# A chunked delta-rule attention kernel with two feed-forward stages: two halves of the key products of every second step made in one go, and the router's ranks moved ahead of the last solve

## The reference

```python
def _attn_ref(q, k, v, beta):              # (4, 8, 768, 48)
    k_n = k / (np.linalg.norm(k, axis=-1, keepdims=True) + 1e-06)
    for t in range(S):
        kt, vt, bt = (k_n[:, :, t], v[:, :, t], beta[:, :, t, None])
        y[:, :, t] = np.einsum('bhd,bhde->bhe', q[:, :, t], state)
        v_old = np.einsum('bhde,bhd->bhe', state, kt)
        state = state + bt[:, :, :, None] * np.einsum('bhd,bhe->bhde', kt, vt - v_old)
def _moe_ref(x, w_in, w_out):              # x (3072, 384), w_in (384, 2048)
    h = x @ w_in
    return (h * (1.0 / (1.0 + np.exp(-h)))) @ w_out
def _moe2_ref(x, w_skip, w_gate, w1, w2):  # 8 experts of 384 x 1024 x 384
    do_compute = x @ w_skip > 0            # the other rows keep x
    e_idx = np.argmax(x @ w_gate, axis=1)  # one expert per row, with gate gate_w
    out = x + gate_w * (relu(x @ w1[e_idx]) @ w2[e_idx])
```

## Time and profile before

| | |
|---|---|
| median of 3 runs | 836.79 us (836.32 to 839.62) |
| the profiled execution | 835.71 us, span on the core 834.0 us |
| PE busy | 793.1 us (95%) |
| DVE / ACT / POOL busy | 569.0 / 369.1 / 112.6 us |

### The profile page before, as it was taken

One profiled execution on the slowest core, in us unless ns is written; L12 is line 12 of the kernel. 1 busy time (PEld: TensorE's weight loads), 2 busy tenths in 40 slices (PEclk: granted clock), 3 DMA queues, 4 the chain that ended last, 5 costly groups with the idle time before them and its releaser, 6 DMA issues.

```text
span 834.0 us, 29247 instructions
## 1 busy us (share of the span) xinstructions
PE 793.1 (95%) x12158; PEld 724.2 (87%) x12159; DVE 569.0 (68%) x1504; ACT 369.1 (44%) x1042; POOL 112.6 (14%) x281
## 2 busy tenths in 40 slices
PE   5978999999999999999999999999999989999994
PEld 3557888899989999889999999999999989999993
DVE  6967887878578685777777677654323667767751
ACT  3722443434435353443434535343543556666641
POOL 1000000001010010101002010000103054344441
PEclk9989999999999999999999999999999999999998
DMA  8743112121211223112220211211023546655610
GB/s 271 219 160 123 46 53 66 60 89 48 92 48 40 91 65 97 42 50 87 66 91 22 66 47 66 64 41 47 32 86 118 186 133 208 198 191 184 188 32 14
DMA packets 46649, 79.75 MB, mean 96 GB/s; under 512 B 5680, under 2 KB 35082, under 8 KB 46144
## 3 DMA queue, kind: packets, MB, share of 16 engines
q1 hardware_dynamic: 43104, 73.07, 27.1%
q0 software_dynamic: 3424, 4.93, 1.9%
HBM read 67.05 MB, written 13.19 MB: 96 GB/s over the span
## 4 chain that ended last, share of the span: by engine, by line
issue 79%; POOL 9%; DMA 6%; POOLq 2%; PE 2%; DVE 1%; ACT 0%; SPq 0%
DMA id_table<-token,slot 5%; POOL idle L680 3%; POOL kq_t L735 2%; POOL id_table L725 2%; PE psum L980 1%; POOL ids_all L731 1%; DMA id_table<-x_sb 1%; POOL out L790 1%; DMA kd<-kq 1%; POOLq L509 0%; POOLq L510 0%; PE psum L836 0%; POOLq L757 0%; POOL token L718 0%; PE psum L981 0%
## 5 line engine op out<-in xcount | busy, mean ns | idle before, releaser
L1014 PE MATMUL psum<-xt_hi,w_hi 128*128 128x256 f32 x768 | 226.3, 295 | 5.3 <-issue 2.7
L1015 PE MATMUL psum<-xt_lo,w_hi 128*128 128x256 f32 x768 | 217.5, 283 | 0.0
L1016 PE MATMUL psum<-xt_hi,w_lo 128*128 128x256 f32 x768 | 217.2, 283 | 0.0
L1190 ACT ACTIVATE h_raw<-psum 128x256 f32<-128x256 f32 x192 | 73.6, 384 | 311.0 <-PE psum L1016 309.3
L1449 DVE TENSOR_TENSOR h_lo<-h_raw,h_hi 128x256 fp32r<-128x256 f32 x192 | 81.4, 424 | 160.2 <-ACT h_hi L1191 159.4
L1014 PEld LDWEIGHTS psum<-xt_hi,w_hi 128*128 128x128 f32 x768 | 145.3, 189 | 14.5 <-issue 8.8
L1016 PEld LDWEIGHTS psum<-xt_hi,w_lo 128*128 128x128 f32 x768 | 146.3, 190 | 0.0
L1015 PEld LDWEIGHTS psum<-xt_lo,w_hi 128*128 128x128 f32 x768 | 145.8, 190 | 0.0
L1038 PE MATMUL psum<-w_hi,h_hi 128*128 128x394 f32 x384 | 138.6, 361 | 1.1 <-DVE h_lo L1449 1.1
L1040 PE MATMUL psum<-w_hi,h_lo 128*128 128x394 f32 x384 | 131.2, 342 | 0.0
L1039 PE MATMUL psum<-w_lo,h_hi 128*128 128x394 f32 x384 | 131.0, 341 | 0.0
(11 more groups left out here) (183 smaller groups left out, 1121.8 us busy)
## 6 DMA issues: line engine op xcount, KB each, us to landing
kq_t<-kq SPq DMA_DIRECT2D x24, 512.0 KB, 3.6
bp<-moe_w SPq DMA_DIRECT2D x24, 512.0 KB, 4.5
kv_t<-kv SPq DMA_DIRECT2D x24, 384.0 KB, 3.1
bp<-moe_w SPq DMA_DIRECT2D x24, 384.0 KB, 4.2
kd<-kq SPq DMA_DIRECT2D x20, 256.0 KB, 3.3
x_table<-x_sb SPq DMA_DIRECT2D x13, 392.0 KB, 2.8
out<-x_sb SPq DMA_DIRECT2D x12, 384.0 KB, 3.1
bp<-moe_w_in SPq DMA_DIRECT2D x6, 512.0 KB, 6.0
```

The costliest lines, as they stand in the source:

```text
L1014: m(out, hi, x_hi, start=first, stop=False)
L1015: m(out, hi, x_lo, start=False, stop=False)
L1016: return m(out, lo, x_hi, start=False, stop=last)
L1190: a_.activation(h_raw[i % 2][:, :], up_ps[i % 2][:, 0:G2], ACT.Silu)
```

## The change

Four things are done, for steps and periods behind the first ones:

- `gram(t, 0)` of odd steps t from 5 on writes banks 6 and 7 (the new entries of `GRAM_BANK`), `gram(t, 1)` still banks 4 and 5, and both are issued one right after the other in slot 28 (before: slots 27 and 30). The gram waits for both `keep` of its period on DVE (`xt_lo_ready`), since those read banks 6 and 7. Reads of the next period wait for the masks of the first half (`r_free`). The masks stay in slots 28 and 30.
- The ranks go to bank 4, columns 384 to 407, and are issued in slot 21 ahead of the last solve (before: slot 28, bank 6); `place` goes from slot 29 to slot 22 on DVE, and waits until ACT has copied that solve out of bank 4. `update` of the even step waits for `place` (`slot_ready`). The last two ranks stay as they were.
- `scales` of step 2p + 3 goes from slot 31 to slot 25 on DVE.
- `USED` is changed to fit, and so `lanes` are spread over the slots in another way.

```diff
@@ -187,6 +187,8 @@
 
 
         GRAM_BANK = {(0, 1): 6, (1, 0): 2, (1, 1): 6, (2, 0): 2, (2, 1): 2, (3, 0): 2}
+
+        GRAM_BANK.update({(t, 0): 6 for t in range(5, T, 2)})
         GRAM_PAIRS = (0, 3), (1, 2)
 
         def gram_ps(t, h):
@@ -216,7 +218,12 @@
 
         score_row = x2_sb[:, :, :].rearrange("p a x -> p (a x)")[:, E * N // P:E * N // P + F // TURN]
         score_ps = psum[:, 0, :].rearrange("p (i j e) -> p i j e", j=TURN, e=Q)[:, :, :, 0:RW]
-        rank_ps = psum[:, 6, 0:3 * E].rearrange("p (a e) -> p a e", a=3)
+        def rank_ps(p):
+
+
+            at = psum[:, 4, HD:HD + 3 * E] if p < NP - 2 else psum[:, 6, 0:3 * E]
+            return at.rearrange("p (a e) -> p a e", a=3)
+
         r_ps = [psum[:, 6 + u, 0:HD] for u in range(2)]
         y_ps = [x.rearrange("p (k c) -> p k c", k=KD) for x in r_ps]
         s_ps = [psum[:, 4 + u, 0:HD] for u in range(2)]
@@ -343,14 +350,14 @@
 
         CHAIN = {0: ("read", 0), 3: ("solve", 0), 6: ("carry", 1), 9: ("solve", 1), 12: ("carry", 2), 15: ("solve", 2),
                  18: ("carry", 3), 21: ("solve", 3), 24: ("update", 0), 26: ("keep", 0)}
-        GRAM_AT = {7: (2, 0), 19: (2, 1), 25: (3, 0), 28: (3, 1)}, {6: (2, 0), 12: (2, 1), 27: (3, 0), 30: (3, 1)}
+        GRAM_AT = {7: (2, 0), 19: (2, 1), 25: (3, 0), 28: (3, 1)}, {6: (2, 0), 12: (2, 1), 28: (3, 0), 30: (3, 1)}
         MASK_AT = {14: (2, 0), 20: (2, 1), 28: (3, 0), 33: (3, 1)}
-        SCALES_AT = {27: 2, 31: 3}, {16: 2, 31: 3}
+        SCALES_AT = {27: 2, 31: 3}, {16: 2, 25: 3}
 
 
         FIRST_AT = {1: 0, 8: 1, 28: 2}
         SPLIT_AT = {17: 0, 19: 1, 21: 2, 23: 3, 25: 4, 29: 5, 31: 6}
-        USED = {0: 10, 6: 18, 7: 10, 12: 18, 13: 10, 16: 11, 18: 10, 19: 4, 24: 14, 26: 11, 27: 16, 28: 3, 29: 10, 30: 16, 31: 11, 10: 13}
+        USED = {0: 10, 6: 18, 7: 10, 12: 18, 13: 10, 16: 11, 18: 10, 19: 4, 22: 10, 24: 14, 25: 11, 26: 11, 28: 16, 30: 16, 31: 5, 10: 13}
 
         def spare(g, z):
             room = max(1, 16 - 4 * (z % 2 == 0) - USED.get(z % SLOTS, 0))
@@ -423,6 +430,8 @@
                     g, z = p // 2, SLOTS * (p % 2) + x
                     if p < NP and x in CHAIN:
                         name, b = CHAIN[x]
+                        if name == "solve" and b == 3 and p >= 2:
+                            s["rank"](p - 2)
                         for t in pair:
                             s[name](t, b)
                         if name == "solve" and b == 3:
@@ -434,7 +443,11 @@
                     if x in GRAM_AT[p > 0]:
                         n, a = GRAM_AT[p > 0][x]
                         if 2 * p + n < T:
-                            s["gram"](2 * p + n, a)
+                            if p == 0 or n == 2:
+                                s["gram"](2 * p + n, a)
+                            elif a == 0:
+                                for e in range(2):
+                                    s["gram"](2 * p + n, e)
                             if p:
                                 s["mask"](2 * p + n, a)
                     if g == 0 and z in MASK_AT:
@@ -469,9 +482,10 @@
                             s["x2"](p - 2)
                         if x == ((15, 10)[p % 2] if p < NP else 4):
                             s["choose"](p - 2)
-                        if x == (28 if p < NP else 5):
-                            s["rank"](p - 2)
-                        if x == (29 if p < NP else 6):
+                        if x == (22 if p < NP else 5):
+                            if p == NP:
+                                s["rank"](p - 2)
+                        if x == (22 if p < NP else 6):
                             s["place"](p - 2)
                     if p == NP and x in FIRST_AT:
                         s["first"](FIRST_AT[x])
@@ -859,7 +873,13 @@
                             pe.wait_ge(state_ready[u], state_count(2 * p + 2))
                         else:
                             pe.wait_ge(u_copied[u], 4 * p + 1 + a)
-                    pe.wait_ge(bp_ready, H * t + HP * a)
+
+                    if t % 2 and t >= 5:
+                        if a == 0:
+                            pe.wait_ge(xt_lo_ready, t - 1)
+                        pe.wait_ge(bp_ready, H * t)
+                    else:
+                        pe.wait_ge(bp_ready, H * t + HP * a)
 
 
                 for c in range(TURN):
@@ -875,8 +895,8 @@
 
 
                 after(pe, xt_lo_ready, t - 1)
-                if t % 2 == 0:
-                    after(pe, slot_ready, t // 2 - 2)
+                if t >= 4:
+                    pe.wait_ge(bp_ready, H * (t // 2 * 2 + 1) + HP)
 
             def read(t, b):
 
@@ -946,6 +966,9 @@
 
                 u = t % 2
                 pe.wait_ge(u_copied[u], 4 * (t // 2) + 4)
+
+                if u == 0:
+                    after(pe, slot_ready, t // 2 - 1)
                 if ends_row(t):
                     return
                 for h in range(H):
@@ -1044,12 +1067,18 @@
             def rank_of(p):
 
                 pe.wait_ge(chosen_ready, p + 1)
-                pe.wait_ge(xt_lo_ready, min(2 * p + 5, T - 1))
-                m(rank_ps[:, 0, :], before_bf, chosen_bf[:, 0, :], start=True, stop=True)
-                m(rank_ps[:, 1, :], before_bf, chosen_bf[:, 1, :], start=True, stop=False)
-                m(rank_ps[:, 1, :], ones_bf[:, :], chosen_bf[:, 0, :], start=False, stop=True)
-                m(rank_ps[:, 2, :], ones_bf[:, :], chosen_bf[:, 0, :], start=True, stop=False)
-                m(rank_ps[:, 2, :], ones_bf[:, :], chosen_bf[:, 1, :], start=False, stop=True).then_inc(rank_done, 1)
+                if p < NP - 2:
+                    pe.wait_ge(u_copied[0], 4 * (p + 2) + 3)
+                    if p % 2 and (p + 5) // 2 < NQ:
+                        pe.wait_ge(diag_out, diag_count((p + 5) // 2, 0))
+                else:
+                    pe.wait_ge(xt_lo_ready, T - 1)
+                ranks = rank_ps(p)
+                m(ranks[:, 0, :], before_bf, chosen_bf[:, 0, :], start=True, stop=True)
+                m(ranks[:, 1, :], before_bf, chosen_bf[:, 1, :], start=True, stop=False)
+                m(ranks[:, 1, :], ones_bf[:, :], chosen_bf[:, 0, :], start=False, stop=True)
+                m(ranks[:, 2, :], ones_bf[:, :], chosen_bf[:, 0, :], start=True, stop=False)
+                m(ranks[:, 2, :], ones_bf[:, :], chosen_bf[:, 1, :], start=False, stop=True).then_inc(rank_done, 1)
 
             def first(n):
 
@@ -1497,8 +1526,12 @@
                     dve.wait_ge(place_step, n[0] + n[1])
 
                 dve.wait_ge(rank_done, p + 1)
-                then(d.tensor_tensor(rank[:, :, :], both_a(next_slot[:, :]), rank_ps[:, 0:2, :], ALU.add))
-                then(d.tensor_tensor(next_slot[:, :], next_slot[:, :], rank_ps[:, 2, :], ALU.add))
+
+                if p < NP - 2:
+                    dve.wait_ge(u_copied[0], 4 * (p + 2) + 4)
+                ranks = rank_ps(p)
+                then(d.tensor_tensor(rank[:, :, :], both_a(next_slot[:, :]), ranks[:, 0:2, :], ALU.add))
+                then(d.tensor_tensor(next_slot[:, :], next_slot[:, :], ranks[:, 2, :], ALU.add))
                 then(d.tensor_tensor(rank[:, :, :], rank[:, :, :], chosen[:, :, :], ALU.mult))
                 d.tensor_scalar(taken, taken, -float(NOWHERE), float(NOWHERE), ALU.mult, ALU.add)
                 then(d.tensor_reduce(slot_f, rank[:, :, :], AX.X, ALU.add))
```

## The result

The change makes the kernel slower: the medians of 13 runs of each are 842.3 and 837.8 us, 4.5 us apart, and the ratio on record (it is not the quotient of the two medians, which would be 1.0054) is 1.0072, 95% interval 1.0056 to 1.0088. A second comparison gave 1.0091 (1.0066 to 1.0117). The forecast was 839.7 us, 0.35% slower, which it counted as the same; above 841.0 it counted as slower. 842.3 lies inside its range of 833.7 to 843.5, but outside the 837.5 to 841.5 of its own case: the kernel is slower, by one and a half times (medians) to twice (ratio) what was forecast.

The account below looks back on a forecast made before the run. The prediction took PE's own instruction stream to bound periods 1 to 10. Savings of 3.0 us against waits of 2.2, 0.6 and 3.1 gave +2.9 us on the 836.8 median: 839.7 us, range 833.7 to 843.5.

Parts of the forecast that it names:

- PE's stream sets the end: Periods 1 to 10: a microsecond taken from PE is won in full, one that PE waits is lost in full.
- Second gram half, 2.2 us: PE, odd steps 5 to 23: a half following another saves 0.22 us per step, ten times, 2.2 us.
- Ranks, 0.8 us: PE, periods 2 to 11: ranks ahead of the solve save 0.08 us each, 0.8 us in all.
- PE waits for `keep`, 2.2 us: Slot 28: merged halves wait for DVE's `keep`, 0.1 us over even periods, 0.36 per odd one, 0.6 in period 1; 2.2 us.
- The transpose, 0.6 us: Periods 3, 5, 7, 9: PE waits 0.15 us each for the `lo` behind DVE's transpose in slot 28; 0.6 us.
- The scales' loads, 3.1 us: Slot 25: `kv_t` loads landing late delay DVE, `keep` and PE one for one; 3.1 us, bounds 0 and 8.
- Nothing for the rest: `place`, moved lanes, SP's loads, POOL's DMAs and the tail were taken to cost 0.
- `place` and `update`: Slot 22: `place` ends 2 us before `update` starts, cost 0; the rival that `update` waits had 4%, 844.7 us.
- the loads decide: Rival, 19%: late loads hold DVE, `keep` and both halves; over 4 us from a 3.5 us mean landing, up to 844.6 us.
- the loads were late: Refers to the rival that loads come in time for slot 25's scales: sum -0.2 us, 836.6 us; 22%.
- both gates closed: Refers to the rival that neither gate closes, `keep` coming before PE: whole gain remains, 833.8 us; 12%.
- the four waits of the earlier trace: Rival, 8%: DVE's new order also removes PE's four waits for DVE, 1.6 us, giving 831.6 us.

Follow-up runs that it names:

- the two runs on one chip: The changed kernel with its transposes in slot 29, once with the odd steps' scales in slot 25 (842.96 us), once with them in 31 (835.30 us).
- the runs with the same work in 25: Changed kernel, odd steps' scales back in slot 31, two same-size DVE multiplications that wait for no load in slot 25; ratio 1.0025 to the kernel before.
- The second shifted run: Changed kernel with 96 matmuls of the first group done twice, so instruction fetches stand 192 PE instructions earlier; ratio 1.0101 to the kernel before.
- 48 instructions at 4 us: Changed kernel with 24 matmuls of the very first group done twice, 48 more PE instructions; ratio 1.0021 to the kernel before.
- either run with the fetches 48 instructions earlier: 24 first-group matmuls done twice, on the changed kernel (1.0021) and on it with odd steps' scales and transposes in slot 31 (0.9936); ratios to the kernel before.

## Why the prediction was right and wrong

- **PE's stream sets the end: right.** In the two runs on one chip that differ in the scales' slot alone, the gates wait 6.7 us less and the stretch is 6.9 shorter.
- **Second gram half, 2.2 us: 1.6.** Two lone halves took 0.60 each and left by an edge of 0.10 each; the pair takes 1.24 and leaves by one. The entry edge is 0.09 as taken (0.27 behind `down`, whose usual distance is 0.18; 0.21 behind `up`, 0.12). So of the two edges' 0.19, the join itself takes back 0.04 and 0.15 to 0.16 is left; the 0.22 had hoped for more than both edges.
- **Ranks, 0.8 us: 1.1 in the trace of the ranks alone.** Right in kind and nearly in size.
- **PE waits for `keep`, 2.2 us: 2.7.** 0.08 where I had 0.02, 0.41 for 0.36, 0.71 for 0.6. `keep` ends 0.10 later behind the scales than I added up (2.41 us from the start of `lo`, not 2.31), the signal takes 0.10 and not 0.05, and PE's undisturbed arrival is 0.10 later than I had it (7.24 from the start of `update`, not 7.14), since I left out its entry edge.
- **The transpose, 0.6 us: 1.7.** 0.31 for 0.15 in each of four periods, and 0.10 more at the matmul behind it. The difference of two long sums (4.65 against 4.52) carried an error as large as itself.
- **The scales' loads, 3.1 us: 4.5 in the trace.** This is the step that failed, and the largest miss in the sum. Its mechanism was right, its size not. DVE is ready for the scales 3.14 us after the issue in every period, and what the ten landings have beyond that adds to 4.5, the same as 7.2 less the 2.7 above; the runs with the same work in 25 say 4.2 to 5.8. The same count over the ten odd steps of the kernel before gives 3.7 (3.9 over the 3.1 that I used). I had that figure and took 3.1, halfway to the 2.4 of all loads together, because "which are late may be chance". It was not: the late ones stand in the same periods run after run and move when the instruction fetches are shifted. The rest of the miss is mostly period 4, 3.1 us before and 4.65 here. That one stays open, since a fetch begins 2.6 to 2.7 us after the issue in both traces. In any case the late loads were half to two thirds of the loss and could be had for nothing, two slots later.
- **Nothing for the rest: wrong by 1.1 us**, the half of slot 6 (0.8, cause open) and the diagonals (0.3, a few tenths of which differ between two traces of one kernel).
- **`place` and `update`: right**; no wait in any trace.
- **The rivals.** The case "the loads decide" was the one that came: a gate sum of 7.2 against the 5.3 of the forecast. Its words were that from a mean landing of 3.5 on the loads cost over 4 us; the mean was 3.5, the cost 4.5. It had 19%, though the ten odd loads of the kernel before already had a mean of 3.4. The other rivals fell: the loads were late, both gates closed, `update` did not wait, and the four waits of the earlier trace rows did not go (PE waits eight times for `lo` in the first list above). No rival said that the early scales would cost this without the join.
- **The rule weighed there.** The Trainium skill (DMA: Bandwidth & Descriptors, Rules for kernel authors) has a DMA's semaphore waited on late. The runs bear it out: 1.0072 and 1.0091 with the wait in slot 25, 1.0000 in slot 27. The same page's fit (Anatomy of one DMA), by which the prediction estimated 2.9 us for a load, is given for DMAs issued from GpSimd; these are issued from SP. The undisturbed ones took 2.7 to 3.2, so the estimate comes near them all the same, and it says nothing of the late ones.

The sum as forecast was -3.0 + 2.2 + 0.6 + 3.1 = +2.9; as measured in the traces -2.7 + 2.7 + 1.7 + 4.5 + 1.1 = +7.3, of the +7.4 of the stretch.

## What to carry to other kernels

Joining work on the bounding engine sets a gate: both halves now wait for whatever the later one needed. The gate alone cost nothing here (0.9999 with the scales in 31). What stands ahead of it on the releasing engine is what costs, and it costs with another gate too (1.0065 with the ranks behind `keep` and no join). So move that work behind; the scales cost 8 us ahead of the gate, the transpose 1.7 ahead of `lo`, and neither anything that the traces show in slot 31. A wait for a load with next to no cover (here 3.14 us against a median landing of 3.1) is not costed by the median; if late landings come in the same places run after run, ask what else is on the queues there.

## What the hardware showed that was not expected

- A 16 KB instruction fetch that begins 1.0 to 1.8 us after the issue of a 384 KB load goes with a landing 3.8 to 4.9 us after the issue (21 loads) instead of 2.7 to 3.2, and the late landings moved when the fetches were shifted. The Trainium skill (Runtime: NRT & Kernel Launch, Instruction fetch mechanics) says that instructions come in blocks of 16 KiB, 256 of them, over a DMA queue of the sequencer's own, and calls the cost of crossing a block mostly hidden; the 256 in my expectation are from there. The second shifted run agrees with the blocks in periods 3 and 6: the fetch went from 0.9 us ahead of the issue to 0.8 and 0.6 behind it, where 64 instructions or about 2 us later was expected. The runs disagree with "hidden": 48 instructions at 4 us took the whole kernel from 1.0072 and 1.0091 to 1.0021.
- Bursts of small matmuls stop at places that hang on the fetches: groups of 64 that take 0.69 us stopped for 0.1 to 1.3 us on the way, within a few matmuls of the same place in run after run, not once in either run with the fetches 48 instructions earlier, and in two other groups with them 192 earlier. That the burst runs out of fetched instructions there is argued, not shown.
